# Second expert weights loaded as runs of four rows per partition, with the inner units renumbered to match

## Chip, cores and metric

The kernel runs on one core of one Trainium2 chip. The metric is the time of one execution in microseconds of the device (us). The trace is one execution taken by the hardware profiler; its times are those of that execution.

## What is computed

Three layers follow each other: a gated recurrent attention (8 heads of 40, 768 steps, batch 4), a mixture of 8 experts in which each of the 3072 tokens goes to its best expert, and a gated dense layer. The change lies in the middle one, cut here to its core:

```python
def _moe_ref(x, w_gate, w_output_gate, w1, w2):
    # x: 3072 x 320, w1: 8 x 320 x 1024, w2: 8 x 1024 x 320
    e_idx = np.argmax(x @ w_gate, axis=1)
    ...
    for e in range(E):
        mask = e_idx == e
        h = np.maximum(x[mask] @ w1[e], 0.0)
        ye = h @ w2[e]
        out[mask] = gate_w[mask, None] * eom[mask, e, None] * ye
```

The 1024 inner units of `h` are summed over in `h @ w2[e]`. Any numbering of them gives the same sum, as long as the columns of `w1[e]` and the rows of `w2[e]` are taken in the same numbering.

## The kernel before

**Stages.** The attention runs from the start of the span to about 165 us and scatters its rows by expert into `x_by_expert`. The expert stage runs from 189 us to 453 us. The dense stage takes the rest.

**Tiles of the expert stage.** There are 19 tiles: `NFULL` = 12 tiles of 256 tokens (`TE`), then `NHALF` = 7 tiles of 128 tokens (`TS`). Which expert a tile belongs to stands in a table made on the chip, so every tile loads both weights of its expert anew.

**Number format.** Every product is made in three parts. A value is split into a high part, rounded to the fp32r format that TensorE multiplies, and a low part, the rest: ScalarE writes the high part, VectorE the low one. `passes` (lines 1407 to 1414) sums high x high, high x low and low x high for three slices of the 320 inputs. The third slice has 64 rows and carries its low part in partitions 64 to 127, so 8 matmuls make one block instead of 9. All of them stand on line 1413.

**One tile on TensorE** (`e_step`):
- `hidden` (the helper with line 1416 and following) makes the 1024 inner units in 8 blocks of 128, 8 matmuls each, 64 in all. The *weight* side of a matmul (the operand held in the array, 128 columns, loaded by an own LDWEIGHTS instruction) is a slice of `first_hi` or `first_lo`; the side that streams through is `xT_hi` or `xT_lo`, 256 or 128 columns wide. No weight is used twice, so there are as many weight loads as matmuls.
- `x_turn` (line 1405) transposes the next tile's tokens: 6 or 3 transposes.
- `expert_out` (lines 1437 to 1439) makes the output: for each of the 8 blocks f of inner units and each 128 tokens three matmuls that stream 320 columns of `second_hi` or `second_lo`. The held operand is `hT_hi` or `hT_lo`. That is 48 matmuls in a tile of 256 tokens and 24 in one of 128.

**Weights.** SyncE issues the loads. `w1_load` (lines 442 and 444) fills `w1_raw` in two halves of 512 columns. `w2_load` (line 453) fills `w2_raw`, a buffer of 128 partitions x 8 blocks x 320, in two halves of 4 blocks. ScalarE rounds them to `first_hi` (line 719) and `second_hi` (line 725), VectorE subtracts for `first_lo` (lines 1103, 1104) and `second_lo` (line 1111). A buffer of raw weights is loaded again once VectorE is done with it; so the loads of tile j+1 run under the matmuls of tile j. The trace calls both raw buffers `w_raw`, and both weight tensors in memory `w`.

**Order.** Nothing schedules by cost: each engine has its own program, written out by hand, and semaphores join them. Block f of the inner units is columns 128 f to 128 f + 127 of `w1[e]`, and partition p of block f in `w2_raw` is row 128 f + p of `w2[e]`, within each half.

Of the kernel before, what the change touches and what calls it, by code (L numbers as in the profile page):

```python
# [32 lines left out]
P = 128  # L33
# [9 lines left out]
F1 = 1024  # L43
# [29 lines left out]
def build(nc, qk, tok, o_tok, ig, fg, wg, wog, w1, w2, wgv, wou, rms_g, out):  # L73
    with ExitStack() as ctx:
# [6 lines left out]
        def sem(name):  # L81
            return ctx.enter_context(nc.semaphore(name))
# [202 lines left out]
        w2_in = [sem(f"w2_in{i}") for i in range(2)]  # L285
# [50 lines left out]
        w2_flat = w2.rearrange("e k n -> (e k) n")  # L336

        @block.sync
        def _(sp):
# [106 lines left out]
            def w2_load(j, ex):  # L446

                for half in range(2):
                    if not (isinstance(j, int) and j == 0):
                        sp.wait_ge(w2_lo, 4 * j + 2 * half - 2)  # L450
                        sp.sem_inc(sync_turn, 1)
                    f = slice(half * NF1 // 2, (half + 1) * NF1 // 2)
                    sp.dma_start(w2_raw[:, f],
                                 w2_flat[bass.ds(ex * F1 + half * F1 // 2, F1 // 2), :].rearrange("(f p) n -> p f n", p=P)).then_inc(w2_in[half], 16)

            def expert_of(j):
                return sp.value_load(expi[0:1, bass.ds(j, 1)], min_val=0, max_val=E - 1)

            def expert_loads(j, w):
                ex = expert_of(j)  # L460
                x_load(j, w)
                w1_load(j, ex)
                w2_load(j, ex)
# [12 lines left out]
            ex = expert_of(0)  # L476
            w1_load(0, ex)
            sp.wait_ge(zero_rows, 16 * (E + TE // TS))
            for n in range(NY):
                sp.wait_ge(scattered[n], 16 * (NT // NY))  # L480
            x_load(0, TE)
            w2_load(0, ex)
            expert_loads(1, TE)

# [784 lines left out]
        def _(pe):  # L1269
# [138 lines left out]
            def passes(dst, whi_, wlo_, xh, xl):  # L1408

                terms = [(whi_(k), xh(k)) for k in range(KB)] + [(whi_(k), xl(k)) for k in range(KB)]  # L1410
                terms += [(wlo_(k), xh(k)) for k in range(2)]
                for n, (w, x) in enumerate(terms):
                    m = mm(dst, w, x, start=(n == 0), stop=(n == len(terms) - 1))  # L1413
                return m

            def hidden(j, w):
                pe.wait_ge(x_lo, 2 * j + 2)
                for r in range(4):
                    if r % 2 == 0:
                        pe.wait_ge(w1_lo, 4 * j + r + 2)  # L1420
                    for a in range(2):
                        c = slice((2 * r + a) * P, (2 * r + a + 1) * P)
                        m = passes(bank[r][:, a * TE:a * TE + w], lambda k: first_hi[:, k, c], lambda k: first_lo[:, k, c],
                                   lambda k: xT_hi[:, k, 0:w], lambda k: xT_lo[:, k, 0:w])
                    m.then_inc(h_made, 1)
# [19 lines left out]
            def e_step(j, w=TE, w_next=TE):  # L1445
                hidden(j, w)
                x_turn(j + 1, w_next)
                expert_out(j, w)
# [5 lines left out]
            with pe.Fori(NFULL, NTE - 1) as j:  # L1454
                e_step(j, TS, TS)
            hidden(NTE - 1, TS)
            expert_out(NTE - 1, TS)

# [81 lines left out]
```

## Time and profile before

| | us |
|---|---|
| median of 3 runs | 885.36 |
| lowest and highest of them | 883.01, 892.77 |
| the profiled execution | 885.66 |
| its span, first to last instruction | 883.9 |
| expert stage in it, first matmul of line 1413 to the end of the last tile | 189.2 to 453.2 |

The span leaves out 1.8 us at the two ends of the execution. In the rows, `PE` is TensorE's matmuls and `PEld` its weight loads, which run beside the matmuls; the time of one is that from its start to its modelled end, and neighbours overlap, so the spacing of matmuls is read from the starts in the chain, not from the mean. `DVE` is VectorE, `ACT` ScalarE, `SPq` SyncE's queue of DMA issues. `f32` in a form of TensorE stands for fp32r too. `PEclk` is the granted clock of TensorE, 1.00 being 2.4 GHz.

### The profile page before, as it was taken

The numbers are of one execution on the slowest core, as the hardware profiler recorded it, in microseconds if no ns is written. First come the engines' busy times: TensorE is split into PE (matmuls) and PEld (weight loads), VectorE is DVE, ScalarE is ACT, GpSimd is POOL, SyncE is SP. The second block draws the span as 40 slices with busy tenths as digits, with TensorE's granted clock in tenths as the row PEclk, the third lists the DMA queues.
The fourth block names the chain that finished last, engine by engine and source line by source line (L and its number), as shares of the span: only waits on it lengthen the run. The fifth ranks groups of instructions, "written<-read, shape, count | busy, mean of one in ns | idle before, by whom it ended". The sixth has DMA issues, their size and how long they took to land.

```text
span 883.9 us, 17960 instructions
## 1 busy us (share of the span) xinstructions
PE 825.1 (93%) x6231; PEld 733.6 (83%) x6231; DVE 512.2 (58%) x1055; ACT 388.0 (44%) x694; POOL 135.2 (15%) x190
## 2 busy tenths in 40 slices
PE   6999998259999999999958999999999999999997
PEld 3878776149999999999956888888888888888886
DVE  5588867547787877878824354354453453453332
ACT  5554553047767767677722323323323223222221
POOL 3658776400000000000011001001001001000000
PEclk8999999569999999999987999999999999999999
DMA  6677773599889989899911001001001001000000
GB/s 183 158 197 213 215 206 99 179 295 267 263 269 254 293 247 303 237 285 297 291 45 31 1 1 60 1 1 60 0 0 59 0 0 53 6 0 30 1 1 30
DMA packets 84906, 113.36 MB, mean 128 GB/s; under 512 B 11880, under 2 KB 63624, under 8 KB 84856
## 3 DMA queue, kind: packets, MB, share of 16 engines
q1 hardware_dynamic: 80376, 102.22, 40.0%
q0 software_dynamic: 2304, 7.88, 2.8%
q10 hardware_dynamic: 2176, 2.62, 0.9%
q8 instruction: 29, 0.48, 0.2%
q14 instruction: 21, 0.17, 0.1%
HBM read 96.31 MB, written 16.38 MB: 127 GB/s over the span
## 4 chain that ended last, share of the span: by engine, by line
PE 86%; DMA 4%; issue 3%; DVE 2%; POOL 2%; ACT 2%; SPq 1%; ACTq 1%; DVEq 0%; POOLq 0%
PE psum L1413 45%; PE psum L1488 5%; PE psum L1489 5%; PE psum L1490 5%; PE psum L1437 4%; PE psum L1439 4%; PE psum L1438 4%; PE psum L1281 2%; PE psum L1326 2%; PE psum L1349 2%; PE psum L1302 2%; PE psum L1296 1%; PE psum L1340 1%; PE psum L1405 1%; PE psum L1469 1%
## 5 line engine op out<-in xcount | busy, mean ns | idle before, releaser
L1243 DVE TENSOR_TENSOR gated_lo<-gated,gated_hi 128x512 fp32r<-128x512 f32 x72 | 49.8, 692 | 185.1 <-ACT gated_hi L809 185.1
L804 ACT ACTIVATE sigm_sb<-psum 128x512 f32<-128x512 f32 x72 | 43.1, 599 | 257.1 <-PE psum L1413 257.1
L1413 PE MATMUL psum<-nT_hi,w_gv_hi 128*128 128x512 f32 x432 | 125.7, 399 | 2.6 <-DVE nT_lo L1230 2.6
L1413 PE MATMUL psum<-nT_lo,w_gv_hi 128*128 128x512 f32 x432 | 125.1, 398 | 0.0
L641 POOL DMA_INDIRECT c_rows<-y_by_slot,slot_idx x24 | 22.8, 950 | 553.8 <-DMA y_by_slot<-y_tile 283.4
L1413 PEld LDWEIGHTS psum<-nT_lo,w_gv_hi 128*128 128x128 f32 x432 | 81.9, 190 | 20.1
L1413 PEld LDWEIGHTS psum<-nT_hi,w_gv_hi 128*128 128x128 f32 x432 | 79.3, 190 | 17.1 <-DVE nT_lo L1230 2.8
L1413 PE MATMUL psum<-nT_hi,w_gv_lo 128*128 128x512 f32 x288 | 90.8, 397 | 0.0
L1488 PE MATMUL psum<-w_out_hi,gated_hi 128*128 128x320 f32 x288 | 89.8, 312 | 0.0
L1489 PE MATMUL psum<-w_out_lo,gated_hi 128*128 128x320 f32 x288 | 89.1, 309 | 0.0
L1490 PE MATMUL psum<-w_out_hi,gated_lo 128*128 128x320 f32 x288 | 88.9, 309 | 0.0
L1413 PE MATMUL psum<-xT_hi,first_hi 128*128 128x256 f32 (+1 forms) x456 | 78.6, 282 | 2.0 <-DVE xT_lo L1096 2.0
L1437 PE MATMUL psum<-second_hi,hT_hi 128*128 128x320 f32 x248 | 78.2, 315 | 1.1 <-DVE hT_lo L1117 1.1
L1413 PE MATMUL psum<-xT_lo,first_hi 128*128 128x256 f32 (+1 forms) x456 | 78.7, 282 | 0.0
L1439 PE MATMUL psum<-second_hi,hT_lo 128*128 128x320 f32 x248 | 76.6, 309 | 0.0
L1438 PE MATMUL psum<-second_lo,hT_hi 128*128 128x320 f32 x248 | 76.6, 309 | 0.0
L725 ACT ACTIVATE second_hi<-w_raw 128x640 fp32r<-128x640 f32 x76 | 54.3, 738 | 36.1 <-PE psum L1439 33.6
L719 ACT ACTIVATE first_hi<-w_raw 128x1536 fp32r<-128x1536 f32 x38 | 56.6, 1491 | 27.0 <-DMA w_raw<-w 27.0
L1413 PEld LDWEIGHTS psum<-xT_hi,first_hi 128*128 128x128 f32 x456 | 65.8, 193 | 2.4 <-DVE xT_lo L1096 2.4
L1111 DVE TENSOR_TENSOR second_lo<-w_raw,second_hi 128x640 fp32r<-128x640 f32 x76 | 59.3, 822 | 11.9 <-ACT second_hi L725 11.3
L1413 PEld LDWEIGHTS psum<-nT_hi,w_gv_lo 128*128 128x128 f32 x288 | 54.4, 189 | 13.5
L1413 PEld LDWEIGHTS psum<-xT_lo,first_hi 128*128 128x128 f32 x456 | 65.4, 194 | 0.0
(208 smaller groups left out, 1550.8 us busy)
## 6 DMA issues: line engine op xcount, KB each, us to landing
w_raw<-w SPq DMA_DIRECT2D x38, 640.0 KB, 6.6
w_raw<-w SPq DMA_DIRECT2D x38, 512.0 KB, 4.5
w_raw<-w SPq DMA_DIRECT2D x76, 128.0 KB, 4.8
kv_tok<-tok SPq DMA_DIRECT2D x24, 324.0 KB, 6.7
qk_sb<-qk SPq DMA_DIRECT2D x48, 160.0 KB
y_by_slot<-y_tile SPq DMA_DIRECT2D x12, 321.0 KB, 7.0
og_tok<-o_tok SPq DMA_DIRECT2D x24, 160.0 KB, 6.1
x_tile<-x_by_expert SPq DMA_DIRECT2D x12, 320.0 KB, 2.9
```

Of the source, the lines that this page charges most:

```text
L719: nc.scalar.activation(first_hi[:, :, c], w1_raw[:, :, c], ACT.Copy).then_inc(w1_hi, 1)
L725: nc.scalar.activation(second_hi[:, 2 * r:2 * r + 2], w2_raw[:, 2 * r:2 * r + 2], ACT.Copy).then_inc(w2_hi, 1)
L804: nc.scalar.activation(sigm_sb[f % 2][:], bank[2 * (f % 2)][:], ACT.Sigmoid).then_inc(sig_ready, 1)
L1111: dve.tensor_tensor(second_lo[:, f], w2_raw[:, f], second_hi[:, f].bitcast(F32), ALU.subtract).then_inc(w2_lo, 1)
L1243: dve.tensor_tensor(gated_lo[f % 4][:], gated[f % 2][:], gated_hi[f % 4][:].bitcast(F32), ALU.subtract).then_inc(hv_lo, 1)
L1413: m = mm(dst, w, x, start=(n == 0), stop=(n == len(terms) - 1))
L1437: mm(o, hT_hi[:, r, c], second_hi[:, f], start=(f == 0), stop=False)
L1438: mm(o, hT_hi[:, r, c], second_lo[:, f], start=False, stop=False)
L1439: m = mm(o, hT_lo[:, r, c], second_hi[:, f], start=False, stop=(f == NF1 - 1))
L1488: mm(o, gated_hi[f % 4][:, c], w_out_hi[:, f], start=(f == 0), stop=False)
L1489: mm(o, gated_hi[f % 4][:, c], w_out_lo[:, f], start=False, stop=False)
L1490: m = mm(o, gated_lo[f % 4][:, c], w_out_hi[:, f], start=False, stop=(f == NF2 - 1))
```

## The change

Within each half of 512 rows of `w2[e]`, partition p now takes the rows 4p to 4p + 3 instead of the rows p, 128 + p, 256 + p and 384 + p. So the four blocks of a half lie behind one another in memory for each partition: one run of 5120 bytes in place of four of 1280. Block f of a half thus means the inner units 4p + f. To make `h` in the same numbering, the weight slices of `first_hi` and `first_lo` in `hidden` take every fourth column, from the block's number within its half, in place of 128 neighbouring ones.

```diff
@@ w2_load
                     f = slice(half * NF1 // 2, (half + 1) * NF1 // 2)
                     sp.dma_start(w2_raw[:, f],
-                                 w2_flat[bass.ds(ex * F1 + half * F1 // 2, F1 // 2), :].rearrange("(f p) n -> p f n", p=P)).then_inc(w2_in[half], 16)
+                                 w2_flat[bass.ds(ex * F1 + half * F1 // 2, F1 // 2), :].rearrange("(p f) n -> p f n", p=P)).then_inc(w2_in[half], 16)
@@ hidden
                     for a in range(2):
-                        c = slice((2 * r + a) * P, (2 * r + a + 1) * P)
+                        first = r // 2 * (F1 // 2) + 2 * (r % 2) + a
+                        c = slice(first, first + F1 // 2 - 3, 4)
                         m = passes(bank[r][:, a * TE:a * TE + w], lambda k: first_hi[:, k, c], lambda k: first_lo[:, k, c],
                                    lambda k: xT_hi[:, k, 0:w], lambda k: xT_lo[:, k, 0:w])
```

The instructions, their order and their waits are the same on every engine. What differs is how the second weights are read from memory by line 453, and from which addresses the 64 weight loads of `hidden` in each tile read. Behind `hidden` the line numbers are one higher in the changed kernel.

## Rows read from the trace of the kernel before

**Rows 1.** The page, busy time: us, share of the span, instructions.
```profile
span 883.9 us, 17960 instructions
PE 825.1 (93%) x6231; PEld 733.6 (83%) x6231; DVE 512.2 (58%) x1055; ACT 388.0 (44%) x694; POOL 135.2 (15%) x190
```

**Rows 2.** Busy time by stretch: tiles of 256, tiles of 128, first 16 matmuls of line 1413.
```profile
core 0: us, PE busy (x) PEld busy (x) DVE busy (x) ACT busy (x) POOL busy (x), PEclk, DMA share, GB/s
206.31:376.10 169.79, 169.34 (x1300) 169.13 (x1300) 134.59 (x206) 124.20 (x222) 0.00 (x0) 1.00 0.91 267
376.10:453.15 77.05, 76.39 (x631) 75.89 (x630) 58.75 (x97) 53.77 (x105) 0.00 (x0) 1.00 0.84 252
189.19:192.70 3.51, 3.50 (x17) 3.51 (x17) 2.97 (x4) 2.24 (x4) 0.00 (x0) 0.52 1.06 326
```

**Rows 3.** The chain that ended last: start us, length us, what.
```profile
189.19 9.42 PE psum L1413 x64
...
268.50 7.68 PE psum L1413 x64
276.17 0.66 PE psum L1405 x6
276.83 0.15 PE psum L1437
...
283.87 7.68 PE psum L1413 x64
...
398.62 7.10 PE psum L1413 x64
...
409.58 7.10 PE psum L1413 x64
...
489.11 3.73 PE psum L1413 x16
```

**Rows 4.** Who waited for whom, 165 to 470 us, TensorE: total, times, longest.
```profile
PE psum L1405 <- DMA x_tile<-x_by_expert: 20.1, 1, 20.1
PE psum L1437 <- DVE hT_lo L1117: 1.1, 2, 0.7
```

**Rows 5.** Weight loads by shape: busy us, mean ns of one, idle before.
```profile
L1413 PEld LDWEIGHTS psum<-xT_hi,first_hi 128*128 128x128 f32 x456 | 65.8, 193 | 2.4 <-DVE xT_lo L1096 2.4
L1281 PEld LDWEIGHTS psum<-ident,og_tok 128*64 128x64 f32 x384 | 21.2, 140 | 6.7 <-DMA og_tok<-o_tok 3.3 <-issue 1.2
L1349 PEld LDWEIGHTS psum<-prob_T,kv_tok 128*41 128x41 f32 x384 | 21.2, 123 | 4.2 <-issue 4.0
```

**Rows 6.** VectorE's reductions from SBUF by shape: busy us, mean ns of one.
```profile
L928 DVE TENSOR_REDUCE all_logits<-logit_parts 128x16 f32<-128x128 f32 x24 | 8.7, 364 | 0.1
...
L948 DVE TENSOR_REDUCE seen_now<-all_onehot 128x8 f32<-128x32 bf16 x6 | 1.2, 207 | 0.2
...
L941 DVE TENSOR_REDUCE top_logit<-all_logits 128x4 f32<-128x32 f32 x6 | 1.1, 180 | 0.0
...
L1050 DVE TENSOR_REDUCE by_expert<-units_begun 128x8 f32<-128x192 f32 x1 | 0.3, 341 | 0.0
...
L1084 DVE TENSOR_REDUCE by_tile<-tiles_past 128x19 f32<-128x152 f32 x1 | 0.3, 310 | 0.0
...
L1051 DVE TENSOR_REDUCE by_expert<-units_begun 128x8 f32<-128x96 f32 x1 | 0.2, 241 | 0.0
```

**Rows 7.** DMA: queue 1, line 453's issues, and ScalarE's rounding of the second weights.
```profile
q1 hardware_dynamic: 80376, 102.22, 40.0%
...
w_raw<-w SPq DMA_DIRECT2D x38, 640.0 KB, 6.6
...
L725 ACT ACTIVATE second_hi<-w_raw 128x640 fp32r<-128x640 f32 x76 | 54.3, 738 | 36.1 <-PE psum L1439 33.6 <-DMA w_raw<-w 2.4
```

## The prediction

> **What bounds the kernel now.** I read four views. The page first: TensorE is busy 93% of the span and its weight loads 83%, VectorE 58% [rows 1]. The busy time by stretch then shows that in the expert stage, the one that the change touches, TensorE has next to no gap: 169.34 of 169.79 us in the tiles of 256 tokens and 76.39 of 77.05 in those of 128, at the full granted clock of 1.00 [rows 2]. So what this stage takes is the sum of the spacings of its matmuls. These come from the chain that ended last [rows 3]. In a tile of 256 tokens the 64 matmuls of `hidden` take 7.68 us, 120 ns each; the transposes 0.66; and from 276.83 to 283.87 the 48 matmuls of `expert_out` take 7.04 us, 147 ns each. In a tile of 128 tokens the 64 matmuls of `hidden` still take 7.10 us, 111 ns each, though half as many columns stream through. At 2.4 GHz 128 columns are only 53 ns. So there the weight load sets the pace, and in the tile of 256 (107 ns of streaming) load and stream are about equally long. The waits confirm that little else counts: apart from the wait for the stage's first tokens, TensorE waits 1.1 us in two places [rows 4].
>
> What a weight load costs per column is seen from its shapes: 193 ns for 128 columns, 140 for 64, 123 for 41 [rows 5], so (193 - 140)/64 = 0.83 ns a column and about 87 ns that is latency. 128 x 0.83 = 106 ns, which fits the pace of 111. The kernel is bound in `hidden` by how fast TensorE reads weights, and this is what the second half of the change alters.
>
> **The change, part one: the longer runs.** Line 453 issues 38 transfers of 640 KB; each is now 128 runs of 5120 bytes in place of 512 of 1280. All traffic of queue 1 is 102.22 MB in 80376 packets, 1272 bytes each [rows 7], so if a packet is a run, 38 x 384 = 14,592 packets go. The DMA engines are at 0.91 and 0.84 of their time in the two kinds of tile [rows 2], so the transfers may well get shorter. But hardly anybody on the path waits for them: TensorE waits for no weights at all in this stage [rows 4], and ScalarE waits 2.4 us in all for a load in front of `second_hi` [rows 7]. What may be won is what TensorE now loses between its pieces. The stage lasts 263.96 us from 189.19 to 453.15. Its pieces are 9.42 + 11 x 7.68 + 7 x 7.10 for `hidden`, 12 x 7.04 + 7 x 3.52 for `expert_out` (24 x 147 ns in the small tile), and 9.7 for 18 groups of transposes, 262.4 in all. That leaves 1.5 us. Part one is worth 0 to 1.5 us. The first tile's loads are no more: its matmuls wait for tokens, not for the second weights [rows 4].
>
> **Part two: the stepped weight loads.** There are 12 x 64 = 768 in tiles of 256 and 7 x 64 = 448 in tiles of 128. None is added, and no wait. Each now reads 128 elements that lie 16 bytes apart. No weight load of this trace reads with a step, so the price is bounded by the nearest rows.
>
> From below: nothing, if TensorE takes one element in 0.83 ns wherever it lies.
>
> What speaks for a price is VectorE, the only engine in the trace that reads SBUF with such a step [rows 6]. Reductions over neighbouring elements take 241 ns for 96 and 341 for 192, with the same 8 results: 1.04 ns an element and 141 ns fixed; 310 ns for 152 and 180 for 32 lie within 15 ns of that line. Line 928 sums over the heads, an element every 64 bytes: 364 ns for 128, where a dense one would lie between those of 96 and 152, at about 280. That is (364 - 147)/128 = 1.70 ns an element, taking 147 ns as fixed (180 less 32 x 1.04). Line 948 sums one-hot rows of bf16 with a step of 8 elements, which is exactly 16 bytes: 207 ns for 32, or (207 - 147)/32 = 1.88 ns. The second source is TensorE's own streaming: at 2.4 GHz four elements of 4 bytes, 16 bytes, pass in 1.67 ns; measured it is 120 ns for 64 such groups, 1.88, and 3.73 us for 16 matmuls of 512 columns, 233 ns or 1.82 a group [rows 3]. All four figures read as one place of 16 bytes every 1.67 to 1.88 ns. A dense weight load needs one place for four of its elements, at 0.83 ns each, and has time to spare. A stepped one needs a place for each element: 128 x 1.67 = 213 to 128 x 1.88 = 240 ns. I take VectorE's best counted row, 1.70 (24 instances), and 218 ns as the new spacing of all 64 matmuls, in both kinds of tile, since the streams (107 and 53 ns) are shorter and run beside it.
>
> [...]
>
> **The sum.** Tiles of 256: 768 x (218 - 120) ns = 75.3 us. Tiles of 128: 448 x (218 - 111) ns = 47.9 us. Together 123.2. Off that goes what is hidden now: the first tile took 9.42 us because its first 16 matmuls ran in 3.51 us, 219 ns each, at a granted clock of 0.52, the 1.2 GHz level [rows 2, 3]. With 218 ns for the loads that costs nothing more, so 1.7 us of the sum is not new. And the 1.5 us of part one and of the gaps go, because tiles get 6 to 7 us longer and every other engine has more time. 123.2 - 1.7 - 1.5 = 120.0. On the profiled execution of 885.66 us (span 883.9 and 1.8 around it) this gives 1005.7; the median of the runs is 0.3 us lower, so about 1005.5. What is late next is nothing: VectorE and ScalarE work 134.59 and 124.20 us in stretches of 169.79 [rows 2], and these stretches grow by 40%.
>
> The likeliest case's own range: from below, the surcharge of VectorE in ns (84 for 128 elements) put on top of 111 ns, 195 ns: 768 x 75 + 448 x 84 = 95.2 us, less 3.2, or 978. From above 240 ns: 768 x 120 + 448 x 129 = 150.0, less 3.2, or 1032.
>
> **Rivals.**
> - *The step is free.* TensorE reads weights at half the rate at which it streams, so it could have the time to visit a new place for each element. For it: 0.83 ns against the 0.42 ns of streaming. Against: rows 6, at this very step. Then only part one stays, 0 to 1.5 us: about 885, not slower. [...] It decides if a place costs 0.83 ns or less.
> - *The clock falls.* In `hidden` the array would stream for 107 of 218 ns, or 53 of 218. Today 53 of 111 ns holds the clock at 1.00 [rows 2], but 53 of 218 isn't shown anywhere. `hidden` itself would lose nothing (219 ns at the low level [rows 2]), but 320 columns at 1.2 GHz are 267 ns against 147: 24 x 120 ns x 7 = 20 us in small tiles, and in large ones a low stretch of 3.5 us, as at the start of the stage, costs half its length, 1.75 x 12 = 21 us. Up to 41 more: 1006 to 1047.
> - *Load and stream do not overlap* when both ask for a place all the time: 218 + 107 = 325 and 218 + 53 = 271 ns. 768 x 205 + 448 x 160 = 229 us: about 1112. Against: today 106 + 107 ns fit into 120.
> - *The longer runs carry it.* Shorter transfers would have to give more than 8.9 us, and there are 1.5 us of gaps; nearly excluded. That runs of 5120 bytes are cut again and nothing is shortened changes no number here.
>
> **How the numbers follow.** The forecast 0.70, clock 0.12, no overlap 0.04, free step 0.13, longer runs 0.01. The first two fill 978 to 1047; with some width for a price below VectorE's surcharge I give 955 to 1050. That leaves out the free step, most of the no-overlap case and a little more, 0.2 in all. Bounds of 1% are 8.9 us, about what a measurement of this kernel can tell from no change: faster 0.01, same 0.13, slower 0.86.
>
> **What would show it.** In the chain, the pieces of 64 matmuls of `hidden` last 13.9 us (218 x 64) in both kinds of tile, in place of 7.68 and 7.10; the mean of one weight load of that line rises from 193 to about 300 ns, and is unchanged in `expert_out`, whose pieces stay at 7.04 us. The attention and the dense stage keep their lengths. TensorE's share of busy time says nothing, since waiting for weights hides in it. The packets of queue 1 fall to about 65,800. The forecast is wrong if those pieces stay at 7.68 and 7.10 (free step), if they reach 17 us or more (no overlap), or if `expert_out` gets longer at a clock below 1.00.

## Result and the profile after

The changed kernel takes 1035.27 us (median of 4 runs, 1031.37 to 1040.87) against 885.59 us (883.01 to 892.77). The ratio is 1.167, with a 95% interval of 1.162 to 1.173: 17% slower. The forecast was 1005.5 us, with a range of 955 to 1050.

The page of the changed kernel: span, busy time, and further down queue 1 and line 453's transfers.

```profile
span 1032.3 us, 17960 instructions
PE 971.8 (94%) x6231; PEld 881.0 (85%) x6231; DVE 519.1 (50%) x1055; ACT 393.4 (38%) x694; POOL 135.1 (13%) x190
...
q1 hardware_dynamic: 65784, 102.22, 33.5%
...
w_raw<-w SPq DMA_DIRECT2D x38, 640.0 KB, 5.9
```

The instructions are as many as before, and TensorE's busy share is 94% where it was 93% [rows 1]: the 148 us by which the span grew are hidden in "busy". The longer runs are real: 14,592 packets fewer, as worked out. The transfers of 640 KB land in 5.9 us where they took 6.6 [rows 7]; how much of this the runs do is seen below, where each half of the change runs alone. The chain that ended last shows the price; its columns are start, length and what.

```profile
191.38 15.33 PE psum L1413 x64
...
214.41 14.91 PE psum L1413 x64
229.32 0.66 PE psum L1405 x6
237.01 14.91 PE psum L1413 x64
...
462.70 14.89 PE psum L1413 x64
477.59 0.66 PE psum L1405 x3
...
482.63 14.90 PE psum L1413 x64
...
502.81 14.89 PE psum L1413 x64
```

A piece of 64 matmuls of `hidden` now takes 14.9 us in both kinds of tile, 233 ns a matmul, where it took 7.68 and 7.10 us [rows 3]. The period of a large tile is 237.01 - 214.41 = 22.60 us. Less 14.91 and 0.66 that leaves 7.03 us for `expert_out`, as before. In the small tiles a second thing shows: three transposes take 0.66 us instead of 0.35, and the period, 20.18 us from 482.63 to 502.81, leaves 4.6 us for an `expert_out` that took 3.5. This grows from tile to tile: the last `expert_out`, from 599.26 to 604.65 us, takes 5.4. The busy time by stretch says why (the last three columns are granted clock, DMA share, GB/s):

```profile
214.41:462.70 248.29, 248.29 (x1298) 248.29 (x1297) 139.58 (x206) 127.26 (x221) 0.00 (x0) 1.00 0.63 184
462.70:604.65 141.95, 141.82 (x634) 141.56 (x634) 60.87 (x97) 56.61 (x106) 0.00 (x0) 0.66 0.43 135
```

In the large tiles the clock stays at 1.00; in the small ones its mean is 0.66. The low level seen below is 0.50, so the clock lies there for about two thirds of the time. Before, it was 1.00 in small tiles too [rows 2]. And the weight loads themselves, by shape (busy us, mean ns of one), against 193 ns in [rows 5]:

```profile
L1413 PEld LDWEIGHTS psum<-xT_lo,first_hi 128*128 128x128 f32 x456 | 121.0, 329 | 0.0
```

### The profile page after: what moved, and what is told of

Its sections match the earlier page's. It is cut to its first block, busy times and chain, and to the rows that moved or that the text cites. A ratio compares the mean times of both kernels' runs of the same rounds, so it can differ in the third digit from the quotient of the medians.

```text
span 1032.3 us, 17960 instructions
## 1 busy us (share of the span) xinstructions
PE 971.8 (94%) x6231; PEld 881.0 (85%) x6231; DVE 519.1 (50%) x1055; ACT 393.4 (38%) x694; POOL 135.1 (13%) x190
## 4 chain that ended last, share of the span: by engine, by line
PE 82%; POOL 7%; issue 5%; DMA 3%; DVE 1%; ACTq 1%; ACT 1%; SPq 1%; POOLq 0%; DVEq 0%
PE psum L1413 54%; PE psum L1489 4%; PE psum L1490 4%; PE psum L1491 4%; PE psum L1438 4%; PE psum L1439 4%; PE psum L1440 4%; POOL zT L605 2%; POOL prob_T L579 2%; PE psum L1405 1%; POOL x_by_expert L612 1%; PE psum L1470 1%; POOL v_weighted L589 1%; DMA x_by_expert<-zero 1%; POOL faded L597 1%
## 5 line engine op out<-in xcount | busy, mean ns | idle before, releaser
L1413 PE MATMUL psum<-xT_hi,first_hi 128*128 128x256 f32 (+1 forms) x456 | 132.1, 405 | 2.0 <-DVE xT_lo L1096 2.0
L1413 PE MATMUL psum<-xT_lo,first_hi 128*128 128x256 f32 (+1 forms) x456 | 133.0, 408 | 0.0
L1413 PEld LDWEIGHTS psum<-xT_hi,first_hi 128*128 128x128 f32 x456 | 120.7, 329 | 2.4 <-DVE xT_lo L1096 2.4
L1413 PEld LDWEIGHTS psum<-xT_lo,first_hi 128*128 128x128 f32 x456 | 121.0, 329 | 0.0
L1117 DVE SCALAR_TENSOR_TENSOR hT_lo<-psum,hT_hi 128x512 fp32r<-128x512 f32 (+1 forms) x76 | 44.9, 592 | 127.4 <-ACT hT_hi L731 127.0
L731 ACT ACTIVATE hT_hi<-psum 128x512 fp32r<-128x512 f32 (+1 forms) x76 | 39.4, 519 | 173.6 <-PE psum L1413 173.6
L1413 PE MATMUL psum<-xT_hi,first_lo 128*128 128x256 f32 (+1 forms) x304 | 97.6, 408 | 0.0
L1413 PEld LDWEIGHTS psum<-xT_hi,first_lo 128*128 128x128 f32 x304 | 85.5, 329 | 0.0
L1438 PE MATMUL psum<-second_hi,hT_hi 128*128 128x320 f32 x248 | 82.9, 334 | 0.0
L1439 PE MATMUL psum<-second_lo,hT_hi 128*128 128x320 f32 x248 | 80.6, 325 | 0.0
```

Of the source, the lines that this page charges most:

```text
L731: nc.scalar.activation(of_width(hT_hi[:, r], w), of_width(bank[r][:], w), ACT.Relu).then_inc(h_hi, 1)
L1117: dve.scalar_tensor_tensor(out=of_width(hT_lo[:, r], w), in0=of_width(bank[r][:], w), scalar=0.0, in1=of_width(hT_hi[:, r].bitcast(F32), w ...
L1438: mm(o, hT_hi[:, r, c], second_hi[:, f], start=(f == 0), stop=False)
L1439: mm(o, hT_hi[:, r, c], second_lo[:, f], start=False, stop=False)
```

## Experiments

A run named below is compared with the kernel before on the same chip. The theory at this point: TensorE reads SBUF in places of 16 bytes, one in 1.82 ns (233 ns / 128), and a step of 4 columns makes each element a place of its own. The rivals: the runs share in the cost, any step costs, the low clock has another cause.

### One half of the change at a time

Only the runs:

```diff
-                                 w2_flat[...].rearrange("(f p) n -> p f n", p=P)).then_inc(w2_in[half], 16)
+                                 w2_flat[...].rearrange("(p f) n -> p f n", p=P)).then_inc(w2_in[half], 16)
```

> Only the longer runs of line 453; the weight loads of hidden read neighbouring columns as before, so the first layer's units are summed against the wrong rows of the second weights. Theory (the step alone costs): 884 to 886 us, the 64-matmul pieces at 7.68 and 7.10 us, queue 1 at about 65,800 packets with a lower share of the DMA engines. Rival (the longer runs themselves cost time, for instance by landing later): clearly above 890.

Only the step:

```diff
-                        c = slice((2 * r + a) * P, (2 * r + a + 1) * P)
+                        first = r // 2 * (F1 // 2) + 2 * (r % 2) + a
+                        c = slice(first, first + F1 // 2 - 3, 4)
```

> Only the stepped weight loads; the second weights are read from memory as before, so units and rows do not match. Theory: 1035 us within 5, pieces of 14.9 us, as the changed kernel. Rival (part of the cost comes from the runs): between 890 and 1025.

The runs alone: ratio 1.0006 (0.9974 to 1.0037), no difference. Its median, 891.1, looks like more than the expected 886, but that of the kernel before was 887.6 in the same series, and the spread is 9 us in both. The step alone: 1035.7 us, ratio 1.164 (1.159 to 1.169), the whole effect. The chain of the step alone:

```profile
258.86 14.91 PE psum L1413 x64
...
483.05 14.99 PE psum L1413 x64
```

The chain of the runs alone:

```profile
244.97 7.68 PE psum L1413 x64
...
406.00 7.10 PE psum L1413 x64
```

So the gain of 0 to 1.5 us that the longer runs might have had can't be seen in the time, and they do no harm. They don't shorten the transfers by much either: the 640 KB land in 6.4 us (median) with the runs alone and in 6.2 with the step alone, against 6.6 before and 5.9 with both. More of the shortening goes with the longer stage than with the longer runs: in the changed kernel's large tiles the DMA engines are busy for 0.63 of the time, where it was 0.91.

### The size of the step

Steps of 2 and 3. With a step of 2 the renumbering goes with runs of two rows (the diff is against the changed kernel):

```diff
-                    sp.dma_start(w2_raw[:, f],
-                                 w2_flat[...].rearrange("(p f) n -> p f n", p=P)).then_inc(w2_in[half], 16)
+                    sp.dma_start(w2_raw[:, f].rearrange("p (g t) n -> p g (t n)", g=2),
+                                 w2_flat[...].rearrange("(g p t) n -> p g (t n)", g=2, t=2)).then_inc(w2_in[half], 16)
...
-                        first = r // 2 * (F1 // 2) + 2 * (r % 2) + a
-                        c = slice(first, first + F1 // 2 - 3, 4)
+                        first = r * 2 * P + a
+                        c = slice(first, first + 2 * P - 1, 2)
```

> The same renumbering with runs of two rows (2560 bytes) and a step of 2 columns, 8 bytes, so that each 16-byte place holds two of the wanted elements. Theory (one place of 16 bytes takes 1.82 ns = 233/128, elements in it come along): 64 places are 117 ns, so the pace stays at 111 to 120 ns, pieces 7.1 to 7.7 us, 884 to 887 us in all. Rival (any step costs in proportion to the bytes spanned or to the step): 140 ns or more, 64 x 20 ns x 19 tiles = 24 us or more on top, above 909.

The step of 3 is the changed kernel with one line different:

```diff
-                        c = slice(first, first + F1 // 2 - 3, 4)
+                        c = slice(first, first + 3 * P - 2, 3)
```

> Step of 3 columns, 12 bytes, in the first product; units are computed from other columns than they should. Theory (price per 16-byte place): 128 elements lie in 96 places, 96 x 1.82 = 175 ns, pieces 11.2 us in both kinds of tile, about 885 + 768 x 55 ns + 448 x 64 ns = 956 us. Rival A (all steps below 16 bytes are free): pieces 7.1 to 7.7 us and 885 us. Rival B (a step that leaves fewer than two hits on some place costs as much as one hit on each): 233 ns, 1035 us.

Step of 2, a large tile and a small one in the chain:

```profile
239.46 7.67 PE psum L1413 x64
...
378.17 7.48 PE psum L1413 x64
```

Step of 3, the same:

```profile
248.10 11.23 PE psum L1413 x64
...
418.07 12.44 PE psum L1413 x64
```

| step | bytes | places in 128 elements | places x 1.82 ns | spacing in large tiles, ns | in small tiles, ns |
|---|---|---|---|---|---|
| 1 | 4 | 32 | 58 | 120 | 111 |
| 2 | 8 | 64 | 117 | 120 | 117 |
| 3 | 12 | 96 | 175 | 175 | 194 |
| 4 | 16 | 128 | 233 | 233 | 233 |

The price per place hits the spacing within 1 ns wherever nothing else is longer and the clock stays high. Rival "all steps below 16 bytes are free" falls with the 175 ns, and "any step costs", in its form of 140 ns or more, with the 120. One thing these rows can't tell: up to a step of 4 the number of places and the stretch of addresses grow together (32 places and 512 bytes a step), so a price for each 16 bytes spanned would give the same four numbers. With a step of 2 the small tiles pay 64 x 6 ns x 7 = 2.7 us, and the whole is not told from the kernel before: ratio 1.0016 (0.9983 to 1.0050).

The step of 3 took 973.3 us where 956 was expected, because the theory in that form left the clock out. In its small tiles the clock falls (mean 0.71 in the first piece), their pieces last 12.4 to 12.7 us where 11.2 was expected, and the `expert_out` behind them gets longer, as in the changed kernel. Three rows of one small tile, columns start, length:

```profile
454.43 0.69 PE L1413 MATMUL psum<-xT_hi,first_hi 128*128 128x128 f32 x3
454.95 0.69 PE L1413 MATMUL psum<-xT_lo,first_hi 128*128 128x128 f32 x3
...
459.56 0.84 PE L1413 MATMUL psum<-xT_lo,first_hi 128*128 128x128 f32 x3
460.20 0.63 PE L1413 MATMUL psum<-xT_hi,first_lo 128*128 128x128 f32 x2
```

The clock in the stretches around them:

```profile
453.30:457.00 3.70, 3.70 (x23) 3.70 (x23) 3.14 (x5) 1.86 (x5) 0.00 (x0) 1.00 0.86 257
...
461.00:465.00 4.00, 4.00 (x21) 4.00 (x20) 2.34 (x3) 0.38 (x1) 0.00 (x0) 0.50 0.21 81
```

At 1.00 three matmuls take 0.52 us, about 175 ns each; after the fall (0.55 from 457 to 461 us, 0.50 from 461 on) 0.64, 213 each. With a step of 4 it is 233 at either level. One small tile of the changed kernel passes from one to the other in the middle of its piece, and the piece still takes 14.90 us (482.63 above):

```profile
484.00:486.00 2.00, 2.00 (x10) 2.00 (x10) 1.93 (x3) 1.30 (x4) 0.00 (x0) 1.00 0.94 304
490.00:492.00 2.00, 2.00 (x11) 2.00 (x10) 0.43 (x2) 1.76 (x2) 0.00 (x0) 0.50 0.51 201
```

So the place costs the same at both levels, and at 0.50 something else takes 213 ns for a load and 128 columns of stream, which hides the 175 ns of a step of 3 but not the 233 of a step of 4. The three transposes, with dense reads, take 0.66 us there, 220 ns each, where they took 0.35. What in the low level takes the 213 ns, the load or another part of the pair, no run here tells.

### The low clock in the small tiles

The changed kernel, with TensorE made to stream 256 columns in small tiles too:

```diff
-                        m = passes(bank[r][:, a * TE:a * TE + w], ...
-                                   lambda k: xT_hi[:, k, 0:w], lambda k: xT_lo[:, k, 0:w])
+                        m = passes(bank[r][:, a * TE:a * TE + TE], ...
+                                   lambda k: xT_hi[:, k, 0:TE], lambda k: xT_lo[:, k, 0:TE])
```

> The changed kernel, but hidden streams 256 columns in the tiles of 128 tokens too; the upper 128 are left over from earlier tiles and nobody reads their results. Theory (in small tiles the clock falls because little streams per stepped load): with 256 columns the array streams 107 of 233 ns, as in the large tiles, which kept 1.00. The pieces of hidden stay at 14.9 us, expert_out goes back to 3.5 us and the transposes to 0.35, so a small tile takes 18.8 us instead of 19.9 to 20.5 and the kernel 1025 us, 8 to 11 less than the changed one, although TensorE does more. Rival (the low clock in small tiles has another cause, or is harmless): clock still about 0.66 in that stretch, 1035 us.

The step only in large tiles:

```diff
-                        c = slice((2 * r + a) * P, (2 * r + a + 1) * P)
+                        first = r // 2 * (F1 // 2) + 2 * (r % 2) + a
+                        c = slice(first, first + F1 // 2 - 3, 4) if w == TE else slice((2 * r + a) * P, (2 * r + a + 1) * P)
```

> Step of 4 only in the 12 tiles of 256 tokens, with the second weights in the old order (so units and rows do not match there); small tiles as before. Theory: 12 pieces of 14.9 us and 7 of 7.10, granted clock 1.00 throughout the stage, 885 + 11 x 7.23 + 5.9 = 971 us. Rival (the clock also falls behind the large tiles): 980 or more.

The wide stream took 1025.8 us (1.156, 1.151 to 1.161), 9.5 us less than the changed kernel's 1035.3, although 448 matmuls stream twice as much. The two were measured in different series; by the ratios to the kernel before, 1.167 and 1.156, it is about 10 us, and by the stretches of small tiles in the two traces, 141.95 and 130.94 us, 11.0. Its stretch of small tiles and its chain:

```profile
463.06:594.00 130.94, 130.94 (x634) 130.77 (x633) 60.73 (x97) 54.20 (x105) 0.00 (x0) 1.00 0.46 146
```

```profile
481.83 14.91 PE psum L1413 x64
496.73 0.33 PE psum L1405 x3
...
500.59 14.91 PE psum L1413 x64
```

The clock is 1.00, the period 18.76 us. Nothing but the width of the stream was changed, so the clock falls in the small tiles of the changed kernel because of how little streams beside each slow load; with 256 columns beside the same loads it holds. The step in large tiles only took 972.9 us, 971 expected, with pieces of 14.91 and 7.10 us; its small tiles run at 1.00, so behind large tiles nothing lags.

### Does the streamed side pay, and do both share a path?

The kernel before, its streamed operand read with a step of 2 over two slices:

```diff
+            def spread(x, k, w):
+                s = min(k, 1)
+                return x[:, s:s + 2].rearrange("p k t -> p (k t)")[:, 0:2 * w:2]
...
-                                   lambda k: xT_hi[:, k, 0:w], lambda k: xT_lo[:, k, 0:w])
+                                   lambda k: spread(xT_hi, k, w), lambda k: spread(xT_lo, k, w))
```

> The kernel before, weights dense, but what streams in hidden (xT_hi, xT_lo) is read with a step of 2 columns, 8 bytes, across two slices; the first product is computed from other values than it should. Theory (the streaming read pays 1.82 ns per 16-byte place too): 256 columns lie in 128 places, 233 ns, pieces 14.9 us in large tiles; 128 columns in 64 places, 117 ns, pieces 7.5 us in small ones; 885 + 768 x 113 ns + 448 x 6 ns = 975 us. Rival (streaming has time to spare, only weight loads pay): 7.7 and 7.1 us, 885.

The same edit in the changed kernel:

> The changed kernel with the streamed side read with a step of 2 as well, so that in large tiles weight load and stream each need 128 places, and in small ones 128 and 64; the first product is computed from other values than it should. Theory (two readers with a path each): the longer of the two sets the pace, 233 ns in both kinds of tile, 1035 us as the changed kernel. Rival (one path for both): 466 and 350 ns, 29.9 and 22.4 us a piece, 885 + 768 x 346 + 448 x 239 ns = 1258 us or more.

Streamed step alone, 967.8 us:

```profile
257.21 14.52 PE psum L1413 x64
...
468.07 7.44 PE psum L1413 x64
```

Both steps, 1041.4 us:

```profile
259.57 15.16 PE psum L1413 x64
...
465.04 15.03 PE psum L1413 x64
```

The stream pays as well: 227 ns for 128 places (1.77 a place, 3% under the theory, which gave 975 us), 116 for 64. Here each place holds two of the wanted elements, and still the large tile pays almost double, 227 ns for 120: the stream asks for 256 columns, which lie in 64 places when dense and in 128 with a step of 2. With both steps the spacing is 237 and 235 ns, the longer of the two and not their sum, 466 or 350; 2 to 4 ns come on top, and the whole is 6 us above the 1035 expected, within what these two runs can tell. A single path that serves one place in 1.82 ns for both sides is excluded: each side gets its places beside the other.

The small tiles of the last two runs say one thing more of the clock. With a step on the stream, its 128 columns beside dense loads, every 116 ns, ran at 1.00; the same stream beside the stepped loads, every 235 ns, had a mean of 0.67, about as in the changed kernel.

### Is it the number of places, or the stretch of addresses?

Same `spread`, with four neighbouring columns and then four left out; in the second run shifted by two columns:

```diff
-                return x[:, s:s + 2].rearrange("p k t -> p (k t)")[:, 0:2 * w:2]
+                return x[:, s:s + 2].rearrange("p k (g y) -> p (k g) y", y=8)[:, 0:w // 4, 0:4]
```

> The kernel before, weights dense; what streams in hidden is read as 4 neighbouring columns, then 4 left out, each four filling one 16-byte place, so the same 512 (or 256) columns are spanned as with the stream's step of 2, but half the places are touched; the first product is computed from other values than it should. Theory (what counts is the number of places touched): 64 and 32 places, pace 120 and 111 ns, pieces 7.7 and 7.1 us, 885 us. Rival (what counts is the stretch spanned, or any break in the addresses): 227 ns in large tiles, 14.5 us, 968 us.

```diff
-                return x[:, s:s + 2].rearrange("p k (g y) -> p (k g) y", y=8)[:, 0:w // 4, 0:4]
+                return x[:, s:s + 2].rearrange("p k (g y) -> p (k g) y", y=8)[:, 0:w // 4, 2:6]
```

> As the run before, but shifted by two columns, so each four neighbouring columns lie across two 16-byte places; the first product is computed from other values than it should. Theory: 128 and 64 places, as the stream's step of 2: pieces 14.5 us in large and 7.4 us in small tiles, 968 us. Rival (places of 32 bytes or more, or four neighbours come at once wherever they lie): 7.7 and 7.1 us, 885 us.

Aligned fours, 882.3 us (0.998, 0.993 to 1.003), with 118 ns a matmul in large tiles where dense it is 120:

```profile
237.85 7.54 PE psum L1413 x64
...
398.20 7.10 PE psum L1413 x64
```

Fours across two places, 968.3 us (1.093):

```profile
258.15 14.52 PE psum L1413 x64
...
457.68 7.47 PE psum L1413 x64
```

Two columns of shift, 8 bytes, nearly double the time of a large tile's piece. The same stretch is spanned and the same number of elements read; what differs is only in how many aligned 16-byte places they lie. On the streamed side this settles that it is the count of places. On the weight side no run has groups or a step beyond 4; that it is places there too, and not the stretch, is argued from the same price (1.82 ns against 1.77) and not shown.

### Renumbering where the weights are split

Could the runs be had without the step on TensorE? ScalarE and VectorE touch each first weight once, in `w1_high` and `w1_low`. There the columns can be put in block order; the matmuls then read neighbours. With the runs of the changed kernel:

```diff
+        def blocks(x):
+            return x.rearrange("p k (f q) -> p k f q", f=4)
+
+        def raw(x):
+            return x.rearrange("p k (q f) -> p k f q", f=4)
...
-                nc.scalar.activation(first_hi[:, :, c], w1_raw[:, :, c], ACT.Copy).then_inc(w1_hi, 1)
+                nc.scalar.activation(blocks(first_hi[:, :, c]), raw(w1_raw[:, :, c]), ACT.Copy).then_inc(w1_hi, 1)
...
-                dve.tensor_tensor(first_lo[:, :, c], w1_raw[:, 0:2, c], first_hi[:, 0:2, c].bitcast(F32), ALU.subtract).then_inc(w1_lo, 1)
+                dve.tensor_tensor(blocks(first_lo[:, :, c]), raw(w1_raw[:, 0:2, c]), blocks(first_hi[:, 0:2, c].bitcast(F32)), ALU.subtract).then_inc(w1_lo, 1)
```

(and the same for the second subtraction).

> Runs of four rows with the renumbering made where the first weights are split: ScalarE and VectorE read w1_raw with a step of 4 and write first_hi and first_lo block by block, and TensorE reads neighbouring columns. Theory: pieces of hidden at 7.68 and 7.10 us again; ScalarE's line 719 rises from 1.49 us by 0.66 to 0.84 ns x 1536, to 2.5 to 2.8, VectorE's 1103 from 1.22 to 1.9 to 2.1; both still fit into large tiles (VectorE 12.2 + 2.0 of 15.4 us) and just about into small ones (8.4 + 2.0 of 10.96): 884 to 895 us. Rival (a stepped read costs these engines double or more, or the transfers start too late): small tiles get longer than 10.96 us and the kernel 895 to 930.

In the second run both helpers iterate in memory order, so that the reads of `w1_raw` are dense and the writes stepped:

```diff
-            return x.rearrange("p k (f q) -> p k f q", f=4)
+            return x.rearrange("p k (f q) -> p k q f", f=4)
...
-            return x.rearrange("p k (q f) -> p k f q", f=4)
+            return x.rearrange("p k (q f) -> p k q f", f=4)
```

> As the run before, but read in memory order and written with a step: neighbouring elements go 512 bytes apart, and VectorE reads its second operand with that step too. Theory (the price per 16-byte place is one of reading): ScalarE's line 719 stays near 1.49 us, VectorE's 1103 rises as with one stepped read, to about 2.0; 884 to 892 us. Rival (a stepped write costs as much as a stepped read): 719 at 2.5 us or more and the time as with the stepped read or worse.

909.2 us (1.025, 1.020 to 1.030) and 908.9 us (1.024, 1.019 to 1.029). TensorE is whole again, with large tiles' pieces at 7.68 us, but the splitting is slow. Both runs miss their theory (884 to 895 and 884 to 892 us). With stepped reads:

```profile
L725 ACT ACTIVATE first_hi<-w_raw 128x1536 fp32r<-128x1536 f32 x38 | 114.7, 3018 | 23.4 <-DMA w_raw<-w 23.4
L1109 DVE TENSOR_TENSOR first_lo<-w_raw,first_hi 128x1024 fp32r<-128x1024 f32 x38 | 77.0, 2026 | 29.6 <-ACT first_hi L725 29.6
```

With stepped writes:

```profile
L725 ACT ACTIVATE first_hi<-w_raw 128x1536 fp32r<-128x1536 f32 x38 | 114.7, 3022 | 23.0 <-DMA w_raw<-w 23.0
```

ScalarE's rounding goes from 1.49 us to 3.02 either way, 1.0 ns more an element, double. VectorE's subtraction goes from 1.22 to 2.03, 0.8 ns more, as expected. In small tiles the chain now runs through both engines, though with stepped reads neither is busy for more than 44.1 of the 50.4 us from 422.61 on; it passes from one engine to the next. In it the 64 matmuls are broken off and "ACT first_hi L725" of 2.98 us stands in it once a tile, 12.7 us apart (422.61, 435.31, 448.01) where a small tile took 10.96.

```profile
435.31 2.98 ACT first_hi L725
...
448.01 2.98 ACT first_hi L725
```

My expectation of a stepped write near no cost fell: for ScalarE this write, whose elements go 512 bytes apart in groups of four, costs as much as the read with a step of 16 bytes. Whether the distance or the short groups cost there was not tried. No version here beats the kernel before; the one with runs of two equals it.

## Why the prediction was right, and where it was off

- *What bounds.* Held: nothing waited for the second weights, and longer runs brought nothing that shows (the runs alone, 1.0006).
- *Part two, the mechanism.* Held: with a step of 4 each element costs 1.82 ns, what 16 bytes cost in streaming, as VectorE's row of 364 ns and TensorE's own streaming (233 ns for 512 columns) let expect, and the load alone sets the pace in both kinds of tile. That it is aligned places that count is shown on the streamed side.
- *How many wanted elements a place holds.* On the weight side two in each place, the step of 2, keep the dense pace: 120 ns, and 117 for 111 in small tiles. One in each, the step of 4, takes 233. The step of 3 leaves two in one place of three and one in the others; it takes 175 ns in large tiles, what its 96 places cost, so it is neither free nor at the 233 of the other rival. On the streamed side two in each place are not enough: 227 ns for 120.
- *The size.* This is the term that was mis-sized. I took 218 ns, from VectorE's row, though TensorE's own row stood beside it: 233 ns for 512 columns, which are 128 places too. It measured 233. The 15 ns are worth 15 x (768 + 448) = 18.2 us. One of the readings behind it was wrong as well, without effect on the figure: VectorE's 96 elements in 241 ns (line 1051) are not neighbours but every second one of 192, 8 bytes apart. The rows that do read neighbours are 180 ns for 32 (line 941, in groups of eight), 310 for 152 (line 1084) and 341 for 192 (line 1050). The first and the last alone give (341 - 180)/160 = 1.01 ns an element and 148 fixed, with the 310 within 10 ns of that. By this line 96 neighbours would take 244 ns, so the step of 2, with 241, cost VectorE nothing there; and line 928 gives (364 - 148)/128 = 1.69 ns an element, for the 1.70 that was taken.
- *The clock.* I set it beside the forecast as a rival with a chance of 0.12 and 41 us at most; the forecast itself had it at nothing. The small tiles did lose it (mean 0.66), the large ones did not (1.00). The price of a matmul of 320 columns was as reckoned: in the changed kernel the first nine of the `expert_out` from 498.19 us on take 2.40 us, 267 ns each, and the other 15 take 148. It was paid for 7 of the 24 in the first small tile, 9 in the second and 13 in the last, and never for all. In the rows it is worth 10.9 us: 1.9 of transposes (6 x 0.31), 7.2 in the `expert_out` of the first six small tiles, from 0.9 in the first to 1.4 in the sixth, and 1.8 in the last (5.39 us for 3.58). The wide stream gave back 11.0 in its trace.
- *Where the figures in GHz come from.* The profile gives the two levels as 1.00 and 0.50 of full speed and shows no frequency. The prediction reckons with 2.4 and 1.2 GHz, and so with 53 and 107 ns for 128 and 256 columns, 0.42 a column and 1.67 for four. What the traces have for that is the pace at the low level: in the trace of before, from 474.52 to 477.93 us at 0.50, eight matmuls of 512 columns take 3.41 us, 426 ns each or 1.20 columns a ns, which by estimate would be 2.40 at 1.00. Measured at 1.00, 512 columns take 233 ns, 2.20 a ns; at that pace 128 and 256 columns are 58 and 117 ns.
- *The sum, made again.* The stage lasts 604.65 - 191.38 = 413.27 us where it was 263.96, 149.3 more. The pieces of `hidden` give (15.33 - 9.42) + 11 x 7.23 + 7 x 7.80 = 140.0, the clock 10.9, and the gaps of 1.5 went: 149.4. In the forecast's terms it is 120.0 + 18.2 + 10.9, and 0.4 because the first tile still loses that much at the low level. The span grew by 148.4 only: the stage starts 2.2 us later, and what follows it is 3.1 shorter, 2.8 of them in the first 48 matmuls of the dense stage (11.46 us for 14.28), which ran at a granted clock of 1.00 where the mean had been 0.78. That needs no step: with the aligned fours, whose expert stage is as long as before, the same 48 matmuls took 11.47, at 1.00 too.
- *How much of it is luck.* The likeliest case's own range ended at 1032, just under the measured 1035.3. It lies inside 955 to 1050 because the range was widened for the clock. So the range held for a reason that was named, but two misses went the same way, and the forecast of 1005.5 was 30 us low.
- *Free step, no overlap, longer runs.* None of them came. Weight loads and streams overlap even when both step: 237 ns, where they take 233 and 227 apart.

## What to carry to other kernels

Count aligned places of 16 bytes, not elements, for each operand of a matmul: here one cost 1.82 ns on the weight side and 1.77 on the streamed one, and for the streamed one it is shown that places are what counts. With 4-byte elements a step of 2 is nearly free on the weight side (120 ns as when dense, and 117 for 111), since it stays close to the dense load's own pace, and a step of 4 doubles the spacing (233 ns for 120 and 111). On the streamed side a step of 2 already nearly doubles the spacing of 256 columns (227 ns for 120), and so do 8 bytes of misalignment in groups of four (227 for 118). Don't pay for longer DMA runs with steps on an engine that is the bound; here the transfers were hidden, and the 0.2 us each that the runs alone gave was worth nothing, while the step was paid 1216 times. When a change makes weight loads longer and what streams beside them stays the same, look at the granted clock from there on: here it fell to 0.50 for about two thirds of the time (mean 0.66) where 128 columns streamed every 233 ns, and stayed at 1.00 where 256 did, although TensorE was "busy" all the time in both.

## What the runs showed of the hardware that I had not expected

- The price of a place is nearly the same on TensorE's two sides, 1.82 ns for weights and 1.77 for the stream; a weight load with a step of 4 pays it at both clock levels (233 ns at 1.00 and at 0.50). And the two sides hardly disturb each other (237 ns with both, 233 and 227 apart).
- Two wanted elements in a place are enough for the weight side, but not for the stream: 117 to 120 ns against 227.
- Streaming twice as many columns into results that nobody reads made the kernel about 10 us faster, since it held the clock at 1.00.
- A pair of load and 128 columns takes 111 ns dense at 1.00. At 0.50 it took 213 with a step of 3 (175 at 1.00), and 233 with a step of 4 at either.
- For ScalarE a write with 512 bytes between neighbouring elements costs as much as a read with a step of 16 bytes: 3.02 us for 1536 elements, against 1.49 dense.
